# Attention scores of a routed-expert kernel: fp32 matmuls over zero-padded batches, replaced by fp32r parts in all 128 rows

## The reference

```python
scores = scale * np.matmul(q, k.transpose(0, 1, 3, 2))          # [2, 8, 576, 576]
kth = np.partition(scores, -32, axis=-1)[..., -32:-31]
scores = np.where(scores >= kth, scores, -1000000000.0)
attn = np.exp(scores - np.max(scores, axis=-1, keepdims=True))
attn = attn / (np.sum(attn, axis=-1, keepdims=True) + 1e-09)
x = np.matmul(attn, v)                       # -> [1152, 512], heads side by side
h = x @ w_in                                 # w_in [512, 2048]
g = np.maximum(h, 0.0) + alpha * np.minimum(h, 0.0)
x2 = g @ w_out                               # w_out [2048, 512]
logits = x2 @ w_gate + np.log1p(np.exp(x2 @ w_noise)) * noise     # 8 experts, best two
out[mask] += top2_w[mask, k, None] * (np.maximum(x2[mask] @ w1[e], 0.0) @ w2[e])
```

## Time and profile before

| what | value |
|---|---|
| median of 3 runs | 786.88 us (783.84 to 788.19) |
| profiled execution | 786.68 us, span 784.9 us |
| mean granted TensorE clock | 0.965 |
| busy: TensorE, VectorE, ScalarE, GpSimd | 709.1, 545.1, 408.4, 388.9 us |
| score matmuls (L711), 288 records | 93.5 us busy |
| DMA | 96.47 MB |

### The profile page before, as it was taken

How to read it: one execution, slowest core, us unless ns; L and a number is a source line. 1 busy time by engine, 2 the same in 40 slices (tenths; PEclk the granted TensorE clock), 3 DMA queues, 4 the chain that set the end, 5 groups by cost and what they waited for, 6 DMA issues and landing times. The chain is left out here.

```text
span 784.9 us, 13266 instructions
## 1 busy us (share of the span) xinstructions
PE 709.1 (90%) x4484; PEld 537.9 (69%) x4484; DVE 545.1 (69%) x1149; ACT 408.4 (52%) x811; POOL 388.9 (50%) x288
## 2 busy tenths in 40 slices
PE   5666889899999999999999989729999999999993
PEld 2444556476675766757667566519999989999893
DVE  4999999779878798787987804663555545555520
ACT  2443554565766657666575645722535545535511
POOL 0666778476786767867678670730202202112022
PEclk9988999999999999999999999958999999999998
DMA  9593003602204032040310205364267366375322
GB/s 311 231 379 144 15 1 120 231 1 102 75 28 149 1 108 68 27 147 0 107 67 14 95 16 200 146 199 179 82 200 235 102 224 195 124 243 168 115 35 33
DMA packets 29831, 96.47 MB, mean 123 GB/s; under 512 B 5136, under 2 KB 5136, under 8 KB 28176
## 3 DMA queue, kind: packets, MB, share of 16 engines
q1 hardware_dynamic: 25408, 85.96, 30.8%
q0 software_dynamic: 4384, 9.98, 5.7%
HBM read 77.81 MB, written 37.34 MB: 147 GB/s over the span
## 5 line engine op out<-in xcount | busy, mean ns | idle before, releaser
L1232 POOL TENSOR_SCALAR scores<-scores,top 128x576 f32<-128x576 f32 x72 | 127.0, 1764 | 114.6 <-issue 47.7
L330 DVE MAX8 top<-rest 128x8 f32<-128x576 f32 x216 | 152.0, 743 | 0.0
L1323 POOL DMA_INDIRECT out_dram<-ye,xe x24 | 42.8, 1784 | 217.5 <-ACT ye L1174 212.7
L756 PE MATMUL bank<-w_in_sb,x_t 128*128 128x512 f32 x272 | 123.4, 596 | 0.0
L1234 POOL TENSOR_TENSOR expo<-scores,expo 128x576 f32<-128x576 f32 x72 | 107.7, 1496 | 6.0
L336 DVE MATCH_REPLACE8 rest<-top,rest 128x576 f32<-128x576 f32 x144 | 105.5, 738 | 0.0
L711 PE MATMUL ps_scores<-ktr,q 128*128 128x288 f32 x288 | 93.5, 452 | 11.7 <-DMA ktr<-kt_in_dram 4.7
L784 PE MATMUL bank<-w_out_high,g_parts 128*128 128x512 f32 x288 | 102.3, 416 | 1.2 <-DVE g_parts L497 0.7
L929 PE MATMUL bank<-w_hi,he_t 128*128 128x512 f32 x256 | 91.9, 400 | 0.0
L504 DVE TENSOR_TENSOR w_lo<-raw,w_hi 128x1024 fp32r<-128x1024 f32 x64 | 77.9, 1225 | 19.5 <-ACT w_hi L1121 18.6
L330 DVE MAX8 top<-scores 128x8 f32<-128x576 f32 x72 | 50.9, 747 | 50.7 <-POOL expo L1234 30.0
(11 more groups left out here) (164 smaller groups left out, 1305.4 us busy)
## 6 DMA issues: line engine op xcount, KB each, us to landing
raw<-w_dram SPq DMA_DIRECT2D x64, 512.0 KB, 9.3
x_sorted_dram<-x_sorted_dram SPq DMA_DIRECT2D x7, 2570.0 KB, 10.6
q<-qz_dram SPq DMA_DIRECT2D x18, 256.0 KB, 2.7
xe<-x_sorted_dram SPq DMA_DIRECT2D x8, 514.0 KB, 4.8
w_in_sb<-w_in_dram SPq DMA_DIRECT2D x4, 1024.0 KB, 8.5
w_out_raw<-w_out_dram SPq DMA_DIRECT2D x4, 1024.0 KB, 8.4
out_dram<-x_now SPq DMA_DIRECT2D x1, 3584.0 KB, 28.3
x_sorted_dram<-x_now SPq DMA_DIRECT2D x1, 2570.0 KB, 19.1
```

The source lines that it names most:

```text
L330: nc.vector.max(dst, src).then_inc(chain if r < ROUNDS - 1 else dve_top, 1)
L756: mm = pe.matmul(dst, x_t[:, k, :], w_in_sb[:, k, c * 512:(c + 1) * 512], start=(k == 0), stop=(k == MK - 1))
L1232: nc.gpsimd.tensor_scalar(mask, mask, top[:, n % 4, TOPK - 1:TOPK], None, ALU.is_ge).then_inc(pool_mask, 1)
```

## The change

**Scores.** Keys and queries are each split into a high part, rounded to fp32r, and the rest. `k_parts` holds for one head of one batch the high part of its 64 dimensions in partitions 0 to 63 and the rest in 64 to 127. The queries come twice, in both halves of the partitions, as `q_high` and `q_low`. A tile then takes four fp32r matmuls of 128 x 288: per column half `q_high` against `k_parts`, then `q_low` against it, added up in PSUM.

**Who splits.** ScalarE casts (`high_queries` at the end of turns 1 and 5, for the next block; `high_keys`), GpSimd subtracts (`low_queries` at the end of turns 2 and 6; `low_keys`). For the first keys and queries VectorE subtracts too.

**Second batch.** Keys and values of batch 1 no longer lie in memory from the start. There are ten slots for keys and nine for values; head h of batch 1 takes a slot as it comes free, by loads that SP issues from block 3 on.

**Mixed block.** Its tiles need keys of both batches. The usual scores are taken for batch 0, of which 64 rows are copied. A second group, `other_scores`, uses the keys of batch 1, in the same `ps_scores`, and `copy_other` copies the lower 64 rows. These stand in the turns of tiles 28 to 35 (four turns ahead of the tile that they are for), the key casts in 26 to 33 and the key differences in 27 to 34. Blocks 3 and 4 are written out.

```diff
+Q_HIGH_AT, Q_LOW_AT = {1: 0, 5: 1}, {2: 0, 6: 1}
+K_HIGH_AT = {MIXED * HEADS - 6 + h: h for h in range(HEADS)}
+K_LOW_AT = {MIXED * HEADS - 5 + h: h for h in range(HEADS)}
+OTHER_AT = {MIXED * HEADS - 4 + h: h for h in range(HEADS)}
...
             def topk_pair(tile, n, mixed=False):
                 for k in range(2):
                     dve.wait_ge(act_scores, tile + k + 1)
+                    if mixed:
+                        dve.wait_ge(act_other, n + k + 1)
...
+            first_low_keys(0)
+            dve.wait_ge(act_q[0], 1)
+            nc.vector.tensor_tensor(q_low[:, 0:4, :], q_raw[:, 0:4, :], q_high[:, 0:4, :].bitcast(F32),
+                                    ALU.subtract).then_inc(q_ready[0], 1)
+            first_low_keys(1)
             one_block(0, True)
...
+            def second_keys(h):
+                if h >= K_SLOTS - HEADS:
+                    sp.wait_ge(pe_scores, HEADS * MIXED + h - (K_SLOTS - HEADS) + 1)
+                sp.dma_start(k_raw[:, k_slot(1, h), :], kt_in[HEADS + h]).then_inc(k_in_second[h], 16)
+            def second_values(h):
+                if h >= V_SLOTS - HEADS:
+                    sp.wait_ge(pe_pv, HEADS * MIXED + h - (V_SLOTS - HEADS) + 1)
+                to = v[:, v_slot(1, h), :, 0:DIM]
+                sp.dma_start(to[:, 0:KT - 1, :],
+                             v_in[1, h].rearrange("p (k d) -> p k d", k=KT - 1)[:, :, 0:DIM]).then_inc(v_in_second[h], 16)
...
             blank_rows(1)
-            with sp.Fori(3, BLOCKS) as blk:
+            next_queries(3)
+            blank_rows(2)
+            store_x2(1)
+            next_queries(MIXED)
+            blank_rows(3)
+            for h in range(2, 7):
+                second_keys(h)
...
+            def score_parts(h, b):
+                for n in range(2):
+                    for a, part in enumerate((q_high, q_low)):
+                        mm = pe.matmul(ps_scores[:, n, 0:HALF], part[:, h, :],
+                                       k_parts[:, k_slot(b, h), n * HALF:(n + 1) * HALF],
+                                       start=(a == 0), stop=(a == 1))
+                return mm
             def score_tile(tile, h, blk, b):
...
                 wait(pe, act_scores, tile)
-                for n in range(2):
-                    mm = pe.matmul(ps_scores[:, n, 0:HALF], q[:, h, :], ktr[:, h, n * HALF:(n + 1) * HALF],
-                                   start=True, stop=True)
+                if isinstance(tile, int) and tile - 1 - AHEAD in OTHER_AT:
+                    pe.wait_ge(act_other, OTHER_AT[tile - 1 - AHEAD] + 1)
+                score_parts(h, b).then_inc(pe_scores, 1)
+            def other_scores(h):
+                pe.wait_ge(act_k, HEADS + h + 1)
+                pe.wait_ge(k_low, HEADS + h + 1)
+                pe.wait_ge(act_scores, MIXED * HEADS + h + 2)
+                score_parts(h, 1).then_inc(pe_other, 1)
...
+            def copy_other(h):
+                act.wait_ge(pe_other, h + 1)
+                nc.scalar.activation(scores[DIM:, h % SBUFS, :].rearrange("p (a b) -> p a b", a=2),
+                                     ps_scores[DIM:, :, 0:HALF], ACT.Copy, scale=DIM ** -0.5).then_inc(act_other, 1)
+            def high_queries(blk, part):
+                act.wait_ge(q_in[part], 16 * blk + 16)
+                nc.scalar.copy(q_high[:, 4 * part:4 * part + 4, :], q_raw[:, 4 * part:4 * part + 4, :]).then_inc(act_q[part], 1)
+            def high_keys(b, h):
...
+                wait(act, k_low, HEADS * b + h)
+                at = k_slot(b, h)
+                nc.scalar.copy(k_high, k_raw[DIM:, at, :].rearrange("p (a b) -> p a b", b=DIM)).then_inc(act_k_high, 1)
+                nc.scalar.copy(k_parts[0:DIM, at, :], k_raw[0:DIM, at, :]).then_inc(act_k, 1)
...
+            high_keys(0, 0)
+            high_queries(0, 0)
+            high_keys(0, 1)
             for tile in range(AHEAD):
                 copy_scores(tile, tile)
+                high_keys(0, tile + 2)
+                if tile == 1:
+                    high_queries(0, 1)
...
+            def low_keys(b, h):
+                pool.wait_ge(act_k_high, HEADS * b + h + 1)
+                at = k_slot(b, h)
+                nc.gpsimd.tensor_tensor(k_parts[DIM:, at, :].rearrange("p (a b) -> p a b", b=DIM),
+                                        k_raw[DIM:, at, :].rearrange("p (a b) -> p a b", b=DIM),
+                                        k_high.bitcast(F32), ALU.subtract).then_inc(k_low, 1)
+                pool.wait_ge(k_low, HEADS * b + h + 1)
+            def low_queries(blk, part):
+                pool.wait_ge(act_q[part], blk + 1)
+                at = slice(4 * part, 4 * part + 4)
+                nc.gpsimd.tensor_tensor(q_low[:, at, :], q_raw[:, at, :], q_high[:, at, :].bitcast(F32),
+                                        ALU.subtract).then_inc(q_ready[part], 1)
```

184 lines of the change are left out of this document (134 added, 50 removed).

## The result

The changed kernel takes **830.27 us** (median of 4 runs, 824.40 to 830.91) against 786.64 us (4 runs, 783.84 to 788.19): ratio 1.0542, 95% interval 1.0486 to 1.0599. Slower, as forecast, but by 43.6 us where 23.4 were forecast, and outside the range of 792 to 824. The profiled execution took 829.93 us, its span is 828.2.

What follows compares the result with a forecast made beforehand. VectorE bounds the kernel to about 122 us, then TensorE to 422, with 0.4 us slack at tile 7. +8.7 + 17.1 = 25.8, less 1.75 and 0.6, gives 23.4; 786.7 + 23.4 = 810.1, said as 810 us (range 792 to 824).

Steps and rivals of the forecast that it cites:

- Score matmuls: TensorE's scores of each tile: four fp32r matmuls of 288 columns at 133 ns, saving 0.43 us a tile.
- Ring at tile 7: ScalarE and GpSimd's chain to tile 7's product, slack 0.4 us: the query split starts tile 7 1.4 us later each block.
- net per block of -0.35 us: Repeating blocks: 1.4 us lost at tile 7 less 1.75 us regained, so each block 0.35 us shorter.
- -1.75 to block 5's turn 3: After the mixed block, cheaper score tiles regain 1.75 us, bringing the delay from 25.8 to 24.0 us.
- Queries held by a blank copy: Block 2: block 3's queries land late behind blanking, stalling ScalarE, then TensorE; +9.7 us at turn 3's h_transpose, start included.
- The 1.75 us for the low clock: Block 2, h_transpose of turn 2 to that of turn 3: 1.75 us added for TensorE's low clock.
- The start: First tiles: ScalarE's casts delay VectorE's first maximum from 10.83 to about 12.3 us, +1.5 us (0.5 to 4).
- Mixed block: Blocks 3 and 4: second score groups, copies and key splits add 17.1 us by tile 7 of block 4 (+5 to +28).
- the third pair's scores (301.2): Mixed block: VectorE's third pair waits until 301.2, in the repeating block's coordinates, for the copy of other scores 5.
- Tail: Block 8 onward: no query split and an unchanged chain to tile 7, so nothing added.
- Rival 4: fp32r at 288 columns isn't one pass, or the low clock stays through stops: +10 to +15, about 823 us; chance 0.08.
- Rival 1: TensorE stays the bound, so the price per tile decides: -16, 771 us; chance 0.10.

Runs made afterwards that it cites:

- e1: The changed kernel with the second half of the next block's queries cast and subtracted at turns 2 and 3, not 5 and 6, except in the mixed block: 813.05 us.
- e6: The changed kernel with the moves of e1 and e2, its mixed block without second scores, their copies or batch 1's keys: 777.70 us.
- e2: The changed kernel with block 3's queries issued ahead of the blanking copies on SP's queue: 813.93 us.
- e3: The changed kernel with three unused fp32 matmuls at the end of TensorE's turn 6 in blocks 2 to 7: 819.34 us.
- e7: The changed kernel with second groups of scores kept but using batch 0's keys; batch 1's keys neither loaded nor split: 818.82 us.
- e5: The changed kernel with the moves of e1 and e2 together: 800.03 us.
- e11: e5 with the second groups of tiles 29, 31, 33 and 35 and their copies ahead of the x transpose and MLP layers in their turn: 795.08 us.
- e17: e14 plus e9's VectorE subtractions, two keys split in block 2, mixed-block query split at turns 3 and 4, head 1's values and tile 1's score copy earlier: 790.16 us.
- e14: e5 with all eight second groups of scores one turn sooner, each at its old place in the turn: 792.49 us.
- e9: e5 with the low halves of batch 1's keys made on VectorE instead of GpSimd: 802.64 us.

## Why the prediction was right in direction and wrong in size

- **Score matmuls: right.** 0.13 to 0.14 us each for 133 ns forecast, but for the first of a tile. From the start of a tile's last transpose to the operation behind its scores it is 0.64 us (median at full clock), 1.08 before: 0.44 saved for 0.43 forecast. The Trainium skill's rule for a matmul by itself (TensorE: Matmul & The Clock Gate, Back-to-back issue gap), columns / 2.4 plus 2.5 ns, makes it 122; the trace doesn't bear that out at this shape. e1 and e6 let 2.2 of the 3.4 us a block through.
- **Ring at tile 7: mechanism and wait right, its consequence mis-sized.** The step that failed is the net per block of -0.35 us: it took TensorE's speed behind the wait as before. Blocks at clock 1.00 have -0.6 in e2, e3 and e7; the changed kernel has +1.9, +0.5 and +0.9. Two terms fail for the same reason: -1.75 to block 5's turn 3 (measured 0.0; from tile 39 to 40 the clock is 0.77 and it takes 7.5 us, 6.0 in e3 at 1.00), and the 1.75 that the next five score tiles were to take in block 3 (0.8, at 0.96). Together 6.6 us of the 20.
- **Queries held by a blank copy: mechanism right, 3.8 us too small at the h_transpose of turn 3.** The transfer took 13.1 us as forecast. Its issue was put 2.8 us later and came 6.2 later: the ring of block 1 was counted at 1.8 us, and the shift from tile 14 to 16 grew by 3.2 (3.9 to 7.1), with tile 15's transposes at the low clock after a wait of 2.96 us. e1 has the shift at tile 16 at +3.0. The late start adds to it. The 1.75 us for the low clock stood without a working: from the h_transpose of turn 2 to that of turn 3 it was 8.35 us, 2.4 more than the 5.99 without it. e2 shows that the whole stop hangs on SP's order.
- **The start: +1.5 was 3.0.** ScalarE's cast of key 2 waited for its transfer until 11.76 us, which took 9.6 us to land and not 8.1.
- **Mixed block: right in kind, 6.8 us too small.** The price was put at the full width for 64 rows, and was. Between tile 27 and 39 there is what the forecast named (VectorE waits for copies that come one by one). Counted from tile 27, the x transpose of turn 1 stands at +13.8 (12.6 forecast), tile 34 at +17.2 (13.2), tile 39 at +23.9 (17.1). The largest piece, 2.8 us between the x transpose and tile 34, is the step that failed in the ring: TensorE's speed behind a wait. It waits 2.84 us, then takes 8.30 us at the low clock for what e5 does in 5.60 (without its wait for values) at 1.00. The forecast's range named the low clock, its sum left it out. The order that e11 changes makes this place short, but it is not what the forecast's number had wrong: its time for the third pair's scores (301.2) is also about what TensorE's order gives at full speed (an estimate: the x transpose at 295.2, then 4.94 us as in the kernel before, 0.6 for the second scores and 0.65 for their copy, 301.4). In the trace's time 301.2 is 266.0, and VectorE starts at 270.68. The 2.8 us from tile 34 to 39 and the 1.0 ahead of tile 32 I have not followed. Nor is it shown what the whole block would cost at clock 1.00: e3's filler left the clock low in turn 1 of block 4, and e5, where it is up there, has lost 12.6 us by tile 32, not 10.0, and comes to 22.8.
- **Tail: +2.4 for 0.** Kernels with the same tail differ here by as much in their profiled executions (321.4 us from tile 71 to the end in e17, 323.2 in e5, 320.7 before), so it is left open.
- **Rival 4**, a low clock that stays through the stops, was the one that came nearest (823). I gave it 0.08, because the one row with a low clock showed it behind a wait of 3.8 us and returning soon. Rival 1 (TensorE stays the bound) doesn't hold even in e6, where TensorE still waits for tile 7's product in block 5.

## What to carry to other kernels

Split work that is free by load isn't free by place: before putting it into an in-order engine, follow what stands behind it in that turn to the engine that is the bound. e1 and e14 move a few entries of a table and were worth 17 and 8 us. When the bounding engine gets a new short wait in every block, price the wait and also the clock behind it. And when one engine's work is queued behind an operation that waits for this engine, look for the circle in the timelines, not in the sums of waits: those pointed me to GpSimd, where e9 found nothing to gain, and TensorE's order was worth 6 us. Work moved to another engine can close such a circle tighter, as e9's did on VectorE.

## What the runs showed of the hardware that I had not expected

- TensorE's granted clock fell to the lower level at waits of 2.4 us and stayed there for some 6 us (356.1 to 362.7 at 0.50), though it was busy in all of the turns before. The same wait in e7's blocks 5 and 6 left it at the upper level, in its block 7 not. Which of the two happens is not settled by the length of the wait; e3's filler kept it up throughout blocks 5 to 7.
- Operations on 64 partitions cost about what those on 128 do: 649 ns for 64x576 from PSUM on ScalarE against 651 for 128x576, 674 (64x576) against 613 (128x512) for a cast, 1325 (64x576) against 1277 (128x512) for a difference on GpSimd. VectorE takes 756 ns for the 64x576 difference.
- A load of 256 KB issued behind DRAM-to-DRAM copies of 0.77 and 2.57 MB on the same queue took 13.1 us to land; issued ahead of them (e2), 2.9 us.
